# Reordering a fused attention and two-MLP kernel: normalisation, masks and weight splits change places in the queues

## The reference

```
scores = q @ k.T / 8                     # per batch and head, 576 x 576
mask   = 0 <= row - column < 64          # a sliding causal window
attn   = softmax(where(mask, scores, -1e9)) @ v
x      = attn, heads side by side        # 2304 tokens x 512
x      = (sigmoid(x @ w_gate) * (x @ w_val)) @ w_out
out    = ((x @ w_a) * (x @ w_b)) @ w_out2
```

## Time and profile before

| | us |
|---|---|
| median of 3 runs | 974.21 |
| lowest, highest run | 973.34, 974.84 |
| the profiled execution | 973.34 |
| its span, from the first to the last instruction | 971.5 |
| TensorE busy | 946.7 (97%) |
| VectorE busy | 632.8 (65%) |
| ScalarE busy | 479.9 (49%) |
| GpSimd busy | 189.7 (20%) |

### The profile page before, as it was taken

The page is one execution under the profiler, slowest core; times in us unless marked ns, Lnnn a source line. Parts: engine busy times, 40 slices in busy tenths (PEclk is TensorE's granted clock), DMA queues, the critical chain, the costliest instruction groups (busy, mean ns, idle before and its releaser), DMA issues.

```text
span 971.5 us, 16388 instructions
## 1 busy us (share of the span) xinstructions
PE 946.7 (97%) x5988; PEld 871.8 (90%) x5988; DVE 632.8 (65%) x1299; ACT 479.9 (49%) x943; POOL 189.7 (20%) x276
## 2 busy tenths in 40 slices
PE   5699999999999999999999999999999999999998
PEld 4599998888888888888899999999999999999998
DVE  3577877666666656756667657667566768564756
ACT  4577767656666556733344344434344425344233
POOL 3034334232333213325433000000010000010000
PEclk9699999999999999999999999999999999999999
DMA  8739969938867776755594187676688766777662
GB/s 206 169 99 298 285 205 271 268 111 264 242 194 207 244 206 191 240 198 191 188 360 144 55 327 293 254 276 223 249 321 270 274 227 247 270 280 265 226 255 105
DMA packets 150543, 223.38 MB, mean 230 GB/s; under 512 B 84928, under 2 KB 104384, under 8 KB 148160
## 3 DMA queue, kind: packets, MB, share of 16 engines
q1 hardware_dynamic: 135104, 171.99, 54.0%
q0 software_dynamic: 15360, 50.34, 16.0%
HBM read 179.83 MB, written 42.47 MB: 229 GB/s over the span
## 4 chain that ended last, share of the span: by engine, by line
PE 93%; DMA 2%; DVE 2%; SPq 1%; ACT 1%; issue 1%; DVEq 0%; ACTq 0%
PE ps L595 16%; PE ps L597 15%; PE ps L596 15%; PE ps L713 13%; PE ps L715 13%; PE ps L714 13%; PE ps L587 2%; PE ps L575 2%; PE ps L562 2%; DMA out<-ost 1%; PE ps L548 1%; PE ps L545 1%; DMA v_nat<-in_v 1%; SPq L426 0%; SPq L446 0%
## 5 line engine op out<-in xcount | busy, mean ns | idle before, releaser
L595 PE MATMUL ps<-x_hi,gv_hi 128*128 128x512 f32 (+1 forms) x480 | 181.1, 377 | 0.0
L597 PE MATMUL ps<-x_hi,gv_lo 128*128 128x512 f32 (+1 forms) x480 | 177.2, 369 | 0.0
L596 PE MATMUL ps<-x_lo,gv_hi 128*128 128x512 f32 (+1 forms) x480 | 177.0, 369 | 0.0
L713 PE MATMUL ps<-xc,wc 128*128 128x384 f32 x504 | 171.3, 340 | 0.0
L715 PE MATMUL ps<-xc,wc 128*128 128x384 f32 x504 | 170.3, 338 | 0.0
L714 PE MATMUL ps<-xc,wc 128*128 128x384 f32 x504 | 170.2, 338 | 0.0
L1206 DVE TENSOR_TENSOR tt<-ps,tt 128x384 f32<-128x384 f32 x108 | 59.4, 556 | 86.1 <-PE ps L715 85.8
L231 POOL DMA_DIRECT2D w_raw<-in_moe_w_gate x60 | 45.6, 760 | 349.8 <-DVE wo_lo L1102 337.8
L595 PEld LDWEIGHTS ps<-x_hi,gv_hi 128*128 128x128 f32 x480 | 90.7, 189 | 12.2 <-issue 0.7
L597 PEld LDWEIGHTS ps<-x_hi,gv_lo 128*128 128x128 f32 x480 | 90.5, 189 | 11.6
L596 PEld LDWEIGHTS ps<-x_lo,gv_hi 128*128 128x128 f32 x480 | 90.6, 189 | 10.5
(11 more groups left out here) (107 smaller groups left out, 1667.7 us busy)
## 6 DMA issues: line engine op xcount, KB each, us to landing
wc<-wprep SPq DMA_DIRECT2D x54, 1024.0 KB, 6.9
wc<-wprep SPq DMA_DIRECT2D x54, 768.0 KB, 5.7
wprep<-p_out SPq DMA_DIRECT2D x18, 1792.0 KB, 7.1
w_raw<-in_moe_w_gate POOLq DMA_DIRECT2D x60, 256.0 KB, 3.5
w_raw<-in_moe_w_val POOLq DMA_DIRECT2D x60, 256.0 KB, 3.7
w_raw<-in_moe_w_out POOLq DMA_DIRECT2D x60, 256.0 KB, 4.2
v_nat<-in_v SPq DMA_DIRECT2D x64, 128.0 KB, 4.7
k_nat<-in_k SPq DMA_DIRECT2D x40, 128.0 KB, 4.6
```

What stands on the lines that cost most here:

```text
L595: pe.matmul(dst, w_h, m_h, start=first, stop=False)
L596: pe.matmul(dst, w_h, m_l, start=False, stop=False)
L597: return pe.matmul(dst, w_l, m_h, start=False, stop=last)
L713: pe.matmul(dst, w_h, m_h, start=k in (0, 1, 3) and t == 0, stop=False, skip_group_check=True)
```

## The change

Four things change; no instruction's shape does.

1. POOL issues the loads of the first two weight slots without a wait; the third still waits for the third `fill`. SP no longer waits for the fourth `fill` before it loads the first blocks of the second MLP's weights, and the loads of `v` for doubles 1 and 2 stand one place earlier.
2. In the first four doubles, `mix` stands ahead of the next `score` on TensorE; on ScalarE `mix_hi` and `split_first` move forward; on VectorE both halves of a double are normalised in a row, `mix_lo` stands ahead of them, and the pieces of `split_first` move forward.
3. In the chunks, on VectorE, `normalise` moves behind `split_gv` and `unfill`, and `weights_lo` moves ahead of `hidden`.
4. Also there, `mask_and_max` moves behind `hidden` in the steps with f > 0; with f = 0 it stays ahead of it.

```
--- before.py
+++ after.py
@@ -381,7 +381,8 @@
                 pool.tensor_tensor(s4, a12, s2, ALU.subtract).then_inc(p_sums, 1)
 
             for f in range(W_SLOTS):
-                pool.wait_ge(filled, (2, 3, 4)[f])
+                if f == 2:
+                    pool.wait_ge(filled, 3)
                 weight_dmas(pool, f)
             for s in range(W_SLOTS, CHUNKS * STEPS):
                 w_ring(s // STEPS, s % STEPS)
@@ -487,13 +488,12 @@
             load_qk(sp, 1)
             load_v(sp, 0)
             load_qk(sp, 2)
+            load_v(sp, 1)
             load_qk(sp, 3)
-            load_v(sp, 1)
+            load_v(sp, 2)
             load_qk(sp, 4)
-            load_v(sp, 2)
             load_v(sp, 3)
             load_qk(sp, 5)
-            sp.wait_ge(filled, 4)
             load_weights(0)
             load_weights(1)
             for s in range(CHUNKS * STEPS):
@@ -768,12 +768,12 @@
             score(first[1])
             turn(first[0])
             fill(first[3])
-            score(first[2])
             pe.wait_ge(zeros, 2)
             mix(first[0])
+            score(first[2])
             turn(first[1])
+            mix(first[1])
             score(first[3])
-            mix(first[1])
             turn(first[2])
             mix(first[2])
             turn(first[3])
@@ -1016,19 +1016,19 @@
             turned_copy(first[0])
             exps(first[1], 1)
             copy_k(first[3])
+            mix_hi(first[0])
             exps(first[2], 0)
-            mix_hi(first[0])
             turned_copy(first[1])
             exps(first[2], 1)
+            split_first(0)
+            mix_hi(first[1])
             exps(first[3], 0)
-            mix_hi(first[1])
             turned_copy(first[2])
             exps(first[3], 1)
-            split_first(0)
+            split_first(1)
             mix_hi(first[2])
-            split_first(1)
+            split_first(2)
             turned_copy(first[3])
-            split_first(2)
             split_first(3)
             mix_hi(first[3])
 
@@ -1160,20 +1160,23 @@
                         to_mix = None
                     if d and f == 0:
                         unfill(d)
-                    if to_turn:
-                        normalise(to_turn, 0, 2)
-                        to_mix = to_turn
                     if f + 1 < STEPS or c < CHUNKS - 1:
                         split_gv(c, f + 1)
                     if d and f > 0:
                         unfill(d)
+                    if to_turn:
+                        normalise(to_turn, 0, 2)
+                        to_mix = to_turn
                     split_wo(s, f)
-                    if d:
+                    if d and f == 0:
                         mask_and_max(d, 0)
                         mask_and_max(d, 1)
-                    hidden(s, f, w)
                     if prep_at(s - 1) is not None:
                         weights_lo(prep_at(s - 1))
+                    hidden(s, f, w)
+                    if d and f > 0:
+                        mask_and_max(d, 0)
+                        mask_and_max(d, 1)
                     to_turn = d
                     if c == CHUNKS - 1:
                         if f == 4:
@@ -1345,25 +1348,25 @@
             mask_and_max(first[0], 1)
             unfill(first[2])
             normalise(first[0], 0, 1)
+            normalise(first[0], 1, 1)
             mask_and_max(first[1], 0)
-            normalise(first[0], 1, 1)
             mask_and_max(first[1], 1)
             unfill(first[3])
+            mix_lo(first[0])
             normalise(first[1], 0, 1)
+            normalise(first[1], 1, 1)
             mask_and_max(first[2], 0)
-            mix_lo(first[0])
-            normalise(first[1], 1, 1)
             mask_and_max(first[2], 1)
+            mix_lo(first[1])
+            split_first(0)
             normalise(first[2], 0, 1)
+            normalise(first[2], 1, 1)
             mask_and_max(first[3], 0)
-            mix_lo(first[1])
-            normalise(first[2], 1, 1)
             mask_and_max(first[3], 1)
+            split_first(1)
+            mix_lo(first[2])
             normalise(first[3], 0, 1)
-            split_first(0)
-            mix_lo(first[2])
             normalise(first[3], 1, 1)
-            split_first(1)
             split_first(2)
             split_first(3)
             mix_lo(first[3])
```

3 lines of the change are left out of this document (removed).

## The result

The changed kernel takes 1013.49 us (median of 4 runs, 1012.67 to 1014.82) against 973.78 us: ratio 1.041, 95% interval 1.039 to 1.043. It is slower by 40 us, where 14 were forecast and 1001 was the upper end of the range.

The account below looks back on a forecast made before the run. TensorE was taken as the bound, nearly always busy, so new waits add in full: start 2.6 + chunk waits 7.6 + 1.6 + `weights_lo` 2.9 - 0.45 = +14.2 us, 988.4 us; own range 982 to 994, overall 977 to 1001.

Parts of the forecast that it names:

- the chain from `score` to `turn`: In the chunks, `exps`, cast, `split_gv` and `normalise` precede `turn`; in chunk 0 1.4 us new wait per double with f > 0.
- the 0.45 of `v_nat`: One wait of `mix` for a load of `v_nat` in the first MLP; forecast to vanish, winning 0.45 us.
- Order of the first doubles: Before chunk 0, 1.3 us won up to `mix` 1, then lost again: net +1.1 us, bounds -0.5 to +1.5.
- Transfers: At the start, weight slots issued early delay double 2's last `k_nat`: +1.5 us, between 0 and 2.5.
- `normalise` behind `split_gv`: In chunk 0, waits before `turn`: 1.4 us for five doubles with f > 0, 0.6 for f = 0; 7.6 us together.
- POOL's sums: In about 8 of 11 512-column doubles, sums hold up `hidden`'s last operation: 0.2 us wait each, 1.6 us, bounds 0 and 6.
- The Trainium skill's rule: VectorE casts or operations with two SBUF inputs and GpSimd operations reading SBUF block each other for a whole instruction.
- `weights_lo` before `hidden`: New waits before `down(11)`: 0.9 us in chunk 0, 0.5 each in 1 and 2, 0.95 in 3; sum 2.9 us.
- S+13.15: Chunks 1 and 2: time after `score`'s end (S) when `hidden` is done for `down(11)`, against TensorE's arrival at S+12.6.
- the first rival: Chunk 0's 1.4 us waits also bring TensorE's lower clock, 10 to 12 us more: 998 to 1001 us; chance 0.2.

Follow-up runs that it names:

- `p_first_order`: Kernel before with only the new order of the first four doubles, on TensorE, ScalarE and VectorE: 973.42 us, ratio 1.0002.
- `h_first`: Kernel before with the change's TensorE and ScalarE order of the first doubles, but VectorE's first `normalise` unit of doubles 1 to 3 kept ahead of `mix_lo`: 970.79 us.
- `a_sums_wait`: Changed kernel with POOL's sums held back until the last operation of the same step's `hidden` is done, nothing left out: 993.19 us, ratio 1.0210.
- `p_chunks`: Kernel before with VectorE's new order in the chunks alone, start as before: 1007.11 us, ratio 1.0353.
- `c_mask_norm`: Kernel before with `mask_and_max` behind `hidden` and `normalise` behind `split_gv`, `weights_lo` where it was: 1003.51 us, ratio 1.0323.
- `c_no_sums`: Changed kernel with POOL's sums for the second MLP's weights cut to two columns each: 993.82 us, ratio 1.0216.

## Why the prediction was wrong, step by step

The sign was right, and so were the chain from `score` to `turn` and its 1.4 us; the sum was too small by 25 us (988.4 forecast, 1013.5 measured). The 40.9 us of the profile are: 4.9 for the transfers, 1.4 for the order of the first doubles, 7.5 for `normalise` without the sums, 15.1 of idle time by POOL's sums, 3.3 for `weights_lo`, 6.0 for the clock and 3.5 for the 0.2 us beside each wait, less the 0.45 of `v_nat` and 0.4 in the second MLP.

- **Order of the first doubles, +1.1.** Nothing that can be told from zero in the runs; +0.8 in the profile of `p_first_order`, 1.4 in that of the changed kernel (6.3 less 4.9). Right in size, and the intervals between the `mix` are right. The reason given (one unit of `normalise` now behind the casts) fits `h_first` and is not proved by it.
- **Transfers, +1.5, bound 2.5.** Wrong in size: 4.9 in the profile, 4.7 alone. I took the upper bound from rows in which, by the order of the issues, about one slot's weights were ahead, and here it was two. With none ahead the transfer took 3.3 us, with one 4.8, with two 7.5. The 2.4 us between the two rows, counted once for each slot, would have given 4.8; but that would have been luck, for one slot cost 1.5 us of landing, and the second 2.1 to 2.7 on top.
- **`normalise` behind `split_gv`, 1.4 us a double.** Right: 1.46, 1.47 and 1.15 in the changed kernel's doubles without contention, and 1.47 four times in `a_sums_wait`. For the double with f = 0 it was forecast at 0.6 and is 0.49 here, though 0.68 in `p_chunks` and 1.21 in `a_sums_wait`. In the chunks of 512 columns the room was not 0.2 but about 0.45 us, as the waits of 0.83 beside 1.28 us of contention show.
- **POOL's sums, "0.2 us of wait each: 1.6 us, bounds 0 and 6".** This is the step that failed. I held that `hidden` ran ahead of the sums in chunk 0, and that only a part of an operation would be lost later, 0.4 us. The runs show that the sums lengthen `hidden` by 2.3 to 2.4 us in each of two doubles of chunk 0 and of one double each in chunks 1 and 2, and by 1.3 in the seven others of chunks 1 to 3 that have sums (nine in all there, where I had counted about eight). That is 15.1 us of idle time, and with the clock and the 0.2 us beside each wait it is 20 us (993.2 against 1013.5), where I had 1.6. I had the row (1.34 in place of 0.36) and read it as a slow instruction with its own price. But that cast ends 0.2 us after POOL's third sum, and the four longest operations of the changed kernel end 0.4 to 0.6 us after it: what the row shows is an operation that is held until the third of four sums is over. Three sums are 2.1 us long, and an operation that starts just ahead of the first can lose all of it. The upper bound to take was 2.3 us for each of the 13 doubles with f > 0 that have sums, less the room: some 26 us in place of 6.
- **The Trainium skill's rule** (SBUF — State Buffer, SBUF: two separate sides) has whichever of the two starts first keep the shared pair for its whole instruction. The rows agree that the two block each other, and disagree on who wins: the subtraction started 0.34 us before the first sum, by the profile, whose times on POOL are rough, and ended after the third.
- **`weights_lo` before `hidden`, 0.9, 0.5, 0.5, 0.95.** Measured 0.99, 0.75, 0.77, 0.77 us. Right. (By its own terms the sum for chunks 1 and 2 is S+13.05, not S+13.15.)
- **The 0.45 us of `v_nat`** went, as forecast.
- **The clock**, the first rival (0.2), is in the result, but not as told. The waits of up to 1.8 us in the chunks brought no lower clock in any kernel here. The waits of 3.8 us did: in the changed kernel after both, in `p_chunks` and `c_mask_norm` after the second of two. In `c_mask_norm` the two of 2.0 us did so too; those of the changed kernel and of `p_chunks` did not. It is 5 us of the 40 (6 with the longer start), and it follows from the contention: `a_sums_wait` and `c_no_sums` have none in the chunks. Whether a wait of 2 to 4 us brings it is not settled by these runs.

What remains open: when a wait of 2 to 4 us brings the lower clock; why the subtraction, which starts first, is the one that is held; and why the same two slots gave a landing of 6.9 us in one kernel and 7.5 in another.

## What to carry to other kernels

An edit that moves an instruction into a chain also moves what can hold that instruction up into the chain: look for the other engine that runs beside it, and bound the price by the length of that engine's whole run of work, not by one slow row. Count a wait of TensorE a little above its idle time in the profile, 0.2 us here: with 20 waits that is 4 us. When several links of a chain are lengthened, work out the room once for their sum, since edits apart cost 1.7% here and 3.2% together. A load that starts a chain suffers from what is issued ahead of it on another queue as well, here 768 KB or 1.5 MB on POOL's.

## What the runs showed that I had not expected

A VectorE subtraction of two SBUF tensors, 128x384, took 2.88 us in place of 0.56 when POOL's additions began 0.34 us after it, and a cast 1.29 in place of 0.43; beside the same sums the mask operation, which reads PSUM, took no longer. And two weight slots on POOL's queue stretched not only the landing of SP's small transfers (3.3 to 7.5 us) but their issue (0.5 to 2.7 us), so what was queued behind on SP came later as well.
